# An attention and mixer kernel: transfers in another order with more buffers, the 1e-9 as a pair sum, other slots for key tiles and idle transposes

## The chip, the cores and the metric

One Trainium2 chip, of which the kernel uses one core. The metric is the device time in microseconds of one execution; the median of several runs is given. The engines are TensorE (PE; its weight loads are shown as PEld), VectorE (DVE), ScalarE (ACT), GpSimd (POOL), and SyncE (SP), which here only issues transfers. The engines run side by side, each works through its own instructions in order, and they wait for each other through semaphores.

## What is computed

Three stages, all in fp32 (`B, H, S, D = 2, 8, 768, 64`):

```python
# stage 1: attention over a window of 16 and over block summaries (block = 32)
k_sum = k.reshape(B, H, nb, block, D).max(axis=3)
v_sum = v.reshape(B, H, nb, block, D).mean(axis=3)
scores_l = scale * np.matmul(q, k.transpose(0, 1, 3, 2))      # kept where |i - j| < 16
scores_s = scale * np.einsum('bhsd,bhnd->bhsn', q, k_sum) + np.log(block)
a = np.exp(scores_all - np.max(scores_all, axis=-1, keepdims=True))
a = a / (np.sum(a, axis=-1, keepdims=True) + 1e-09)
x = np.matmul(a, np.concatenate([v, v_sum], axis=2))           # then (B, S, H*D)
# stage 2: h = relu(x @ w_in); u, v = halves; v normalised; u * (w_spatial @ v_n + b); @ w_out
# stage 3: h = relu(x @ w_in); conv of 3 taps over S; sigmoid gate; h * gate @ w_out
```

## The kernel before

Attention works on pairs of heads: 8 pairs, `p` = 0 to 7, and each pair in 3 groups of 4 query tiles of 64 (`GP = 3`, `GT = 4`), so `NG = 24` groups. A software pipeline runs over slots `i` = 0 to 28 (`SLOTS`). Every engine has its own loop over `i`; what is done for one group is spread over six slots:

- TensorE in slot `i`: `scores(i)` (L740, 16 small matmuls, waits for the maxima of group i-1, and at a new pair for the key tiles `kw` and for `q`); then the fills of the slot (`dense(u)`); then in slots under 17 without a `vs` fill four idle transposes (L845, they write a bank that nothing reads); then `transpose_probs(i-2)` (L750, waits for `norm_done` and for the `pT` copy of the group before); then `values(i-3)` (L763, at a new pair also waits for `v` and for the block sums in `vw`).
- VectorE: copy of `pT` of group i-3 (L589; for groups with n % 3 == 1 ScalarE does it, L490); in slots with i % 3 == 1 `key_maxima` of the next pair (L566); `x_l` of group i-5 (L597); for group i-1 `rinv`: add 1e-9 (L604), then the reciprocal (L606); for group i the mask, minimum and copy (L617, four pieces).
- ScalarE: `x_h` of group i-4 (L483), the `pT` copy where it is its turn, the four exponentials of group i (L495), whose accumulators write `rsum`, then the copies of the slot's fills.
- GpSimd, loop at L403: normalise group i-1 (L407, waits for `rinv`); `spread_windows` (L385) where i % 3 == 1, `spread_keys` (L377) where i % 3 == 2; then splitting of weights into a high and a low part (L368, L371): `parts` holds 18 such steps, 3 for each of 4 items `wi` and 2 items `wo`, and slots 3 to 16 take one, later ones two.

`key_maxima`, `spread_windows` and `spread_keys` of pair p+1 make the tiles that `scores(3(p+1))` needs.

The fills are units of other work that `fills_at` puts in slots. `("vs", p)` (L804, 24 small matmuls) and `("vp", p)` (L807, 2) make the block sums of `v`: `vs` in slot 3p-1, `vp` in slot 3p; ScalarE copies the result to `vsum`, and `load_sums(p)` spreads it into `vw`, which `values(3p)` reads. From slot 17 on, 14 fills of stage 2 for batch 0 (`("v", 0, m)`, `("u", 0, f, n)`) follow, 12 large matmuls each (`three`, L771 to L773). The first, `("v", 0, 0)`, waits for `wi_split` 8, the last of the 12 steps of the four `wi` items, and for x of batch 0. After the slots the rest of `seq` runs: batch 1, the product W, the spatial matmuls, then stage 3.

All transfers are issued by SyncE in one order written out by hand (L286 to L311): `load_k(p)`, `load_q(p)`, `load_v(p)`, `load_sums(p-1)`, an item (a weight tile, 512 KB) into one of three `stage` buffers. `k` has 2 buffers, `q` 2, `v` 3 (`NVB`). Each load first waits until its buffer is free (`ks_ready`, `win_pool`, `qk_done`, `pv_done`), and holds up what stands behind it.

`overlay` places tensors of different lifetimes in the same space of SBUF.

Of the kernel before, what the change touches and what calls it, by code (L numbers as in the profile page):

```python
# [19 lines left out]
BLOCK, WINDOW, TQ = 32, 16, 64  # L20


def attention_mixer_program(nc, qT_in, kT_in, vw_in, w_in, wsT_in, b_spatial, woT_in, w_in2, cw_in2, w_out2,
                            out):
    fp32 = mybir.dt.float32
# [26 lines left out]
    NVB, NP_, NST = 3, 4, 3  # L52
# [7 lines left out]
    WARM, KEEP = 20, 4  # L60
# [3 lines left out]
    with ctx:  # L64
# [6 lines left out]
        def overlay(name, *lives):  # L71

            found, most = [], 0
            for life in lives:
# [10 lines left out]
        kw, vw, vs_s, vsum, ks, W_h, W_l = overlay(  # L85
            "space_w",
            [("kw", [128, 2, NT, KA], fp32), ("vw", [KA, NVB, NT, 2 * D], fp32), ("vs_s", [128, 2, 2 * D], fp32),
             ("vsum", [128, 2, 2 * D], fp32), ("ks", [128, 2, NB], fp32)],
# [16 lines left out]
        vn0_h, vn0_l, uT0, _, vraw0, wo2_h, wo2_l = overlay(  # L105
            "space_v",
            [("vn0_h", [128, SC6, FH], f32r), ("vn0_l", [128, SC6, FH], f32r), ("uT0", [128, FC, S], fp32)],
            [("at_v0", [128, SC6, FH], fp32), ("vraw0", [128, SC6, FH], fp32)],
            [("wo2_h", [128, GC, DM], f32r), ("wo2_l", [128, GC, DM], f32r)])
        (qT, kT, P, pT, mask, asel, psel, w2_h, w2_l, woT_h, woT_l, g0_h, g0_l, g1_h, g1_l, _, gm0, _, gm1) = overlay(  # L110
            "space_a",
            [("qT", [128, 2, S], fp32), ("kT", [128, 2, S + 2 * WINDOW], fp32), ("P", [128, NP_, GT, KA], fp32), ("pT", [KA, 2, GT * 128], fp32),
# [15 lines left out]
        rsum = sb("rsum", [128, NG * GT], fp32)  # L128
# [14 lines left out]
        q_in = [sem(f"q_in{i}") for i in range(2)]  # L143
# [5 lines left out]
            sem("psel_ready"), sem("eps_ready"))  # L149
        ring_done, ks_ready, win_act, win_pool, kw_ready, vs_ready, vsum_ready = (  # L150
# [26 lines left out]
        for n, i in enumerate((17, 18, 19, 20, 21, 22, 23, 24, 24, 25, 25, 26, 27, 28)):  # L177
            fills_at[i].append(b0[n])
# [13 lines left out]
        def pT_count(n):  # L192

            return (pT_act, n // GP + 1) if n % GP == 1 else (pT_dve, n // GP * (GP - 1) + 1 + n % GP // 2)
# [53 lines left out]
        def _(sp):  # L248
# [6 lines left out]
            def load_q(p):  # L255
                if p >= 2:
                    sp.wait_ge(qk_done, GP * (p - 1))
                sp.dma_start(qT[:, p % 2, :], qT_in[p]).then_inc(q_in[p % 2], 16)
# [26 lines left out]

            load_k(0)  # L286
            load_q(0)
            load_v(0)
            load_k(1)
            load_q(1)  # L290
            load_v(1)
            load_sums(0)
            load_item(0)
            n = 1
            for p in range(2, NP):
# [3 lines left out]
                load_sums(p - 1)  # L299
# [3 lines left out]
            load_sums(NP - 1)  # L303
# [18 lines left out]
        def _(pool):  # L322
# [80 lines left out]
            for i in range(1, NG + 1):  # L403
# [5 lines left out]
                if i % GP == 1 and i // GP + 1 < NP:  # L409
                    spread_windows(i // GP + 1)  # L410
# [522 lines left out]
```

## Time and profile before

| | |
|---|---|
| median of 3 runs | 357.94 us (355.36 to 358.36) |
| the profiled execution | 356.37 us, of it the span 354.6 us |
| mean granted clock of TensorE | 0.995 |
| TensorE busy | 337.8 us, 95% of the span |
| VectorE busy | 212.5 us, 60% |
| ScalarE busy | 125.9 us, 35% |
| GpSimd busy | 113.1 us, 32% |
| chain that ended last, by engine | TensorE 84%, transfers 7%, ScalarE 3%, VectorE 2% |
| transfers | 25.85 MB; `v` 8 x 576 KB, `k` and `q` 8 x 384 KB each, block sums 8 x 144 KB |

The span goes from the first to the last instruction. A granted clock of 1.00 is 2.4 GHz and 0.50 is 1.2 GHz. The busy time of TensorE includes time in which a matmul is in flight behind another, so it is an upper bound of its work; the start of one group of matmuls to the start of the next is the better price.

### The profile page before, as it was taken

The numbers are of one execution on the slowest core, as the hardware profiler recorded it, in microseconds if no ns is written. First come the engines' busy times: TensorE is split into PE (matmuls) and PEld (weight loads), VectorE is DVE, ScalarE is ACT, GpSimd is POOL, SyncE is SP. The second block draws the span as 40 slices with busy tenths as digits, with TensorE's granted clock in tenths as the row PEclk, the third lists the DMA queues.
The fourth block names the chain that finished last, engine by engine and source line by source line (L and its number), as shares of the span: only waits on it lengthen the run. The fifth ranks groups of instructions, "written<-read, shape, count | busy, mean of one in ns | idle before, by whom it ended". The sixth has DMA issues, their size and how long they took to land.

```text
span 354.6 us, 6382 instructions
## 1 busy us (share of the span) xinstructions
PE 337.8 (95%) x2528; PEld 298.2 (84%) x2528; DVE 212.5 (60%) x498; ACT 125.9 (35%) x365; POOL 113.1 (32%) x124
## 2 busy tenths in 40 slices
PE   7859888999999999999999999999999999999996
PEld 6537566777999899888999999988888889999984
DVE  2558788534416992155345994678666557666652
ACT  4746677656434232253111114232222222222212
POOL 5577698822207999600001950000000000000000
PEclk9989999999999999999999999999999999999999
DMA  8696767502201310055000100000000004000004
GB/s 260 187 258 189 236 185 223 186 8 94 104 2 61 89 44 2 0 177 180 0 0 2 59 2 0 1 2 0 0 2 0 0 2 177 0 2 0 3 0 178
DMA packets 10526, 25.85 MB, mean 73 GB/s; under 512 B 1152, under 2 KB 3456, under 8 KB 10496
## 3 DMA queue, kind: packets, MB, share of 16 engines
q1 hardware_dynamic: 10496, 25.44, 23.0%
q8 instruction: 20, 0.33, 0.4%
q14 instruction: 10, 0.08, 0.1%
HBM read 21.11 MB, written 3.15 MB: 68 GB/s over the span
## 4 chain that ended last, share of the span: by engine, by line
PE 84%; DMA 7%; ACT 3%; DVE 2%; issue 1%; SPq 1%; POOL 0%; ACTq 0%; DVEq 0%
PE bank L771 26%; PE bank L773 25%; PE bank L772 25%; DMA kT<-in_k 4%; PE bank L763 3%; DMA vw<-in_vw 3%; ACT P L495 2%; PE bank L750 2%; PE bank L740 2%; PE bank L804 1%; DMA out<-obuf 1%; DVE rinv L604 1%; DVE ks L566 1%; DVE obuf L685 0%; DVE P L617 0%
## 5 line engine op out<-in xcount | busy, mean ns | idle before, releaser
L495 ACT ACTIVATE P<-P,nmax 128x120 f32<-128x120 f32 x96 | 36.7, 384 | 18.8 <-DVE nmax L617 18.7
L773 PE MATMUL bank<-g_h,W_l 128*128 128x384 f32 x128 | 43.0, 336 | 0.0
L772 PE MATMUL bank<-g_l,W_h 128*128 128x384 f32 x128 | 42.9, 335 | 0.0
L771 PE MATMUL bank<-g_h,W_h 128*128 128x384 f32 x128 | 42.9, 335 | 0.0
L773 PE MATMUL bank<-wo_h,hg_l 128*128 128x512 f32 x96 | 38.0, 396 | 0.0
L772 PE MATMUL bank<-wo_l,hg_h 128*128 128x512 f32 x96 | 38.0, 396 | 0.0
L771 PE MATMUL bank<-wo_h,hg_h 128*128 128x512 f32 x96 | 37.9, 395 | 0.0
L407 POOL TENSOR_TENSOR P<-P,rinv 128x480 f32<-128x480 f32 x24 | 23.7, 987 | 32.3 <-DVE rinv L606 32.3
L773 PE MATMUL bank<-wsT_h,vn_l 128*128 128x384 f32 x96 | 32.1, 334 | 0.0
L771 PE MATMUL bank<-wsT_h,vn_h 128*128 128x384 f32 x96 | 32.1, 334 | 0.0
L772 PE MATMUL bank<-wsT_l,vn_h 128*128 128x384 f32 x96 | 32.1, 334 | 0.0
L551 ACT ACTIVATE cbuf<-cbuf 128x768 f32<-128x768 f32 x16 | 13.5, 846 | 49.5 <-DVE cbuf L699 49.5
L542 ACT ACTIVATE hbuf<-bank 128x384 f32<-128x384 f32 x32 | 15.5, 490 | 41.0 <-PE bank L773 40.0
L589 DVE COPY pT<-bank 120x512 f32<-120x512 f32 x16 | 11.0, 690 | 27.3 <-PE bank L750 27.3
L617 DVE CUSTOM_DVE_ANT_0 P<-bank,mask 128x120 f32<-128x120 f32 x96 | 21.5, 278 | 8.1 <-PE bank L740 8.1
L710 DVE TENSOR_TENSOR pbuf<-hbuf,cbuf 128x768 f32<-128x768 f32 x16 | 15.3, 958 | 16.0 <-ACT cbuf L551 16.0
L771 PEld LDWEIGHTS bank<-g_h,W_h 128*128 128x128 f32 x128 | 24.0, 188 | 0.8 <-ACT hbuf L542 0.2
L772 PEld LDWEIGHTS bank<-g_l,W_h 128*128 128x128 f32 x128 | 24.0, 188 | 0.6
L773 PEld LDWEIGHTS bank<-g_h,W_l 128*128 128x128 f32 x128 | 24.0, 188 | 0.0
L524 ACT ACTIVATE g_h<-gm 128x384 fp32r<-128x384 f32 x16 | 8.4, 526 | 43.0 <-DVE gm L675 43.0
L694 DVE TENSOR_SCALAR cbuf<-hbuf,cw 128x768 f32<-128x768 f32 x16 | 9.9, 619 | 22.3 <-ACT hbuf L542 22.3
L771 PE MATMUL bank<-x_h,wi_h 128*128 128x384 f32 x64 | 22.0, 343 | 0.0
(107 smaller groups left out, 782.7 us busy)
## 6 DMA issues: line engine op xcount, KB each, us to landing
vw<-in_vw SPq DMA_DIRECT2D x8, 576.0 KB, 5.8
kT<-in_k SPq DMA_DIRECT2D x8, 384.0 KB, 5.0
qT<-in_q SPq DMA_DIRECT2D x8, 384.0 KB, 5.6
out<-obuf SPq DMA_DIRECT2D x12, 256.0 KB, 2.1
stage<-in_wsT SPq DMA_DIRECT2D x6, 384.0 KB, 3.0
stage<-in_w_in SPq DMA_DIRECT2D x4, 512.0 KB, 5.9
stage<-in_w SPq DMA_DIRECT2D x4, 512.0 KB, 5.0
stage<-in_wo SPq DMA_DIRECT2D x4, 512.0 KB, 3.6
```

What stands on the lines that cost most here:

```text
L407: g.tensor_tensor(out=pi, in0=pi, in1=rinv[:, n * GT:(n + 1) * GT].unsqueeze(2).to_broadcast([128, GT, KA]), op=ALU.mult).then_inc(norm_do ...
L495: a.activation(P[:, i % NP_, j, :], P[:, i % NP_, j, :], ACT.Exp, bias=nmax[:, c:c + 1], scale=-1.0, accum_out=rsum[:, c:c + 1]).then_inc( ...
L542: a.activation(hbuf[:, G % 2, 1 + n * HS:1 + (n + 1) * HS], bank[6 + n][:, 0:HS], ACT.Relu).then_inc(h_ready, 1)
L551: a.activation(cbuf[:, G % 2, :], cbuf[:, G % 2, :], ACT.Sigmoid).then_inc(sig_ready, 1)
L589: vv.tensor_copy(pT[:, n % 2, :], PTB[0:KA, :]).then_inc(pT_dve, 1)
L617: vv.tensor_tensor_reduce(out=P[:, i % NP_, j, :], in0=SC[e][:, h * KA:(h + 1) * KA], in1=mask[:, kind, :], scale=-SCALE, scalar=LARGEST, ...
L694: vv.tensor_scalar(c, h[:, 0:S], tap[0], None, ALU.mult).then_inc(conv_step, 1)
L710: vv.tensor_tensor(out=pbuf[:, :], in0=hbuf[:, G % 2, 1:S + 1], in1=cbuf[:, G % 2, :], op=ALU.mult).then_inc(hg_ready, 1)
L763: ins = t_.matmul(OT[i % 2][e * D:(e + 1) * D, j * TQ:(j + 1) * TQ], vw[:, p % NVB, r * GT + j, e * D:(e + 1) * D], pT[:, i % 2, (4 * e + ...
L771: t_.matmul(dst, lhs[0](c), rhs[0](c), start=first, stop=False)
L772: t_.matmul(dst, lhs[0](c), rhs[1](c), start=False, stop=False)
L773: ins = t_.matmul(dst, lhs[1](c), rhs[0](c), start=False, stop=last)
```

## The change

- `q` gets three buffers (`NQB`), `v` four (`NVB`). `kw` moves to another overlay to make room. The waits of `load_q` and `load_v` follow the new counts.
- SyncE's order: pairs 0 and 1 as before, then item 0, `k`(2), `q`(2), sums(0), item 1, `v`(2); then for p = 1 to 7: `k`(p+2), `v`(p+2), `q`(p+2), sums(p), an item.
- `rsum` becomes a pair for each column; the second is set to 1e-9 once, and `rinv` is made by a `tensor_reduce` over the pair instead of a `tensor_scalar` add.
- `key_maxima` and `spread_windows` of pair p+1 move from slot 3p+1 to 3p, `spread_keys` from 3p+2 to 3p+1 (for p = 0 they stay in slots 1, 1 and 2).
- ScalarE copies `pT` of the groups with n % 3 == 0 instead of 1.
- The splitting steps: none in slots under 2 and in slots 3p, one in other slots under 18, two from slot 18 on.
- The fills of batch 0 start in slot 18 and not 17; there are still 14, the last in slot 28.
- Warm-up transposes 17, not 20; idle transposes 4 in slots 0 to 2, 2 in later slots under 18 without fills, else none.

```diff
     HS = S // 2
-    NVB, NP_, NST = 3, 4, 3
+    NQB, NVB, NP_, NST = 3, 4, 4, 3
...
     QB = 3 * BLOCK // 16
-    WARM, KEEP = 20, 4
+    WARM = 17
     SLOTS = NG + 5
...
         nmax = sb("nmax", [128, NG * GT], fp32)
-        rsum = sb("rsum", [128, NG * GT], fp32)
+
+        rsum = sb("rsum", [128, NG * GT, 2], fp32)
         rinv = sb("rinv", [128, NG * GT], fp32)
...
         b0 = [("v", 0, m) for m in range(SC6)] + [("u", 0, f, n) for f in range(FC) for n in range(2)]
-        for n, i in enumerate((17, 18, 19, 20, 21, 22, 23, 24, 24, 25, 25, 26, 27, 28)):
+        for n, i in enumerate((18, 19, 20, 21, 22, 23, 24, 24, 25, 25, 26, 26, 27, 28)):
             fills_at[i].append(b0[n])
...
-            return (pT_act, n // GP + 1) if n % GP == 1 else (pT_dve, n // GP * (GP - 1) + 1 + n % GP // 2)
+            return (pT_act, n // GP + 1) if n % GP == 0 else (pT_dve, n // GP * (GP - 1) + n % GP)
...
             def load_q(p):
-                if p >= 2:
-                    sp.wait_ge(qk_done, GP * (p - 1))
-                sp.dma_start(qT[:, p % 2, :], qT_in[p]).then_inc(q_in[p % 2], 16)
+                if p >= NQB:
+                    sp.wait_ge(qk_done, GP * (p - NQB + 1))
+                sp.dma_start(qT[:, p % NQB, :], qT_in[p]).then_inc(q_in[p % NQB], 16)
...
-            load_k(0)
-            load_q(0)
-            load_v(0)
-            load_k(1)
-            load_q(1)
-            load_v(1)
-            load_sums(0)
-            load_item(0)
-            n = 1
-            for p in range(2, NP):
+            for p in range(2):
                 load_k(p)
...
                 load_v(p)
-                load_sums(p - 1)
+            load_item(0)
+            load_k(2)
+            load_q(2)
+            load_sums(0)
+            load_item(1)
+            load_v(2)
+            n = 2
+            for p in range(1, NP):
+                if p + 2 < NP:
+                    load_k(p + 2)
+                    load_v(p + 2)
+                    load_q(p + 2)
+                load_sums(p)
                 if n < 6:
...
                     n += 1
-            load_sums(NP - 1)
             sp.dma_start(cw[:, :], cw_in2).then_inc(cw_in, 16)
...
                                 op=ALU.mult).then_inc(norm_done, 1)
-                if i % GP == 1 and i // GP + 1 < NP:
+
+                if i == 1 or i >= GP and i % GP == 0 and i // GP + 1 < NP:
                     spread_windows(i // GP + 1)
-                if i % GP == 2 and i // GP + 1 < NP:
+                elif i == 2 or i >= GP and i % GP == 1 and i // GP + 1 < NP:
                     spread_keys(i // GP + 1)
-                for _ in range(0 if i < 3 else 1 if i < 17 else 2):
+                for _ in range(0 if i < 2 else 2 if i >= 18 else 0 if i % GP == 0 else 1):
                     if parts:
...
                                  ACT.Copy).then_inc(xh_ready, 1)
-                if 3 <= i < NG + 3 and (i - 3) % GP == 1:
+                if 3 <= i < NG + 3 and (i - 3) % GP == 0:
                     n = i - 3
...
                                      bias=nmax[:, c:c + 1], scale=-1.0,
-                                     accum_out=rsum[:, c:c + 1]).then_inc(exp_done, 1)
+                                     accum_out=rsum[:, c, 0:1]).then_inc(exp_done, 1)
                 for u in fills_at[i]:
...
             vv.memset(eps[:, :], 1e-6).then_inc(eps_ready, 1)
+            vv.memset(rsum[:, :, 1:2], 1e-9).then_inc(floor_ready, 1)
...
             for i in range(SLOTS):
-                if 3 <= i < NG + 3 and (i - 3) % GP != 1:
+                if 3 <= i < NG + 3 and (i - 3) % GP != 0:
                     n = i - 3
...
                     vv.tensor_copy(pT[:, n % 2, :], PTB[0:KA, :]).then_inc(pT_dve, 1)
-                if i % GP == 1 and i // GP + 1 < NP:
+                if i == 1 or i >= GP and i % GP == 0 and i // GP + 1 < NP:
                     key_maxima(i // GP + 1)
...
                     dve.wait_ge(exp_done, GT * i)
-                    vv.tensor_scalar(rinv[:, cols], rsum[:, cols], 1e-9, None, ALU.add).then_inc(den_ready, 1)
+                    if i == 1:
+                        dve.wait_ge(floor_ready, 1)
+                    vv.tensor_reduce(out=rinv[:, cols], in_=rsum[:, cols, :], op=ALU.add,
+                                     axis=AX.X).then_inc(den_ready, 1)
                     dve.wait_ge(den_ready, i)
...
                     pe.wait_ge(kw_ready, p + 1)
-                    pe.wait_ge(q_in[p % 2], 16 * (p // 2 + 1))
+                    pe.wait_ge(q_in[p % NQB], 16 * (p // NQB + 1))
                 if i >= 1:
...
                             ins = t_.matmul(SC[e][odd * TQ:(odd + 1) * TQ, h * KA:(h + 1) * KA],
-                                            qT[rows, p % 2, t * TQ:(t + 1) * TQ], kw[rows, p % 2, t, :],
+                                            qT[rows, p % NQB, t * TQ:(t + 1) * TQ], kw[rows, p % 2, t, :],
                                             start=True, stop=True)
...
                     dense(u)
-                if i < 17 and not any(u[0] == "vs" for u in fills_at[i]):
-                    for _ in range(KEEP):
-                        t_.transpose(bank[2][:, 0:128], ident[:, :], ident[:, :])
+                for _ in range(4 if i < 3 else 2 if i < 18 and not fills_at[i] else 0):
+                    t_.transpose(bank[2][:, 0:128], ident[:, :], ident[:, :])
                 if 2 <= i < NG + 2:
...
                 if 3 <= i < NG + 3:

```

## Rows read from the trace of the kernel before

**Rows 1.** Stretches: length, busy PE, PEld, DVE, ACT, POOL, clock, DMA share, GB/s

```profile
61.78:354.60 292.82, 289.49 (x1716) 261.72 (x1712) 171.61 (x298) 86.17 (x195) 67.79 (x59) 1.00 0.13 42
```

**Rows 2.** Chain of waits up to 66 us: start us, duration us, what

```profile
14.82 8.91 DMA vw<-in_vw
23.77 1.51 PE bank L804 x24
...
27.36 0.61 PE bank L740 x16
...
31.79 8.01 DMA kT<-in_k
```

**Rows 3.** Stretches of the attention slots, columns as in rows 1

```profile
2.00:12.00 10.00, 8.06 (x102) 6.46 (x104) 4.04 (x21) 5.06 (x21) 5.96 (x17) 1.00 0.87 273
...
14.00:27.00 13.00, 8.81 (x140) 6.45 (x141) 6.23 (x36) 7.00 (x32) 7.86 (x8) 0.88 0.93 266
27.00:61.00 34.00, 28.73 (x535) 21.54 (x531) 28.11 (x135) 24.93 (x111) 28.10 (x29) 1.00 0.70 208
...
24.00:25.00 1.00, 1.00 (x24) 0.78 (x16) 0.00 (x0) 0.00 (x0) 1.00 (x2) 0.50 1.08 412
```

**Rows 4.** Timeline of TensorE: start us, duration, engine, line, tiles, shape, count

```profile
36.12 0.40 PE L807 MATMUL bank<-vs_s,psel 128*24 128x128 f32 x2
36.45 0.66 PE L845 MATMUL bank<-ident 128*128 128x128 f32 x4
36.94 0.60 PE L750 MATMUL bank<-ident,P 128*120 128x128 f32 x4
37.47 0.69 PE L763 MATMUL bank<-pT,vw 120*64 120x64 f32 x16
38.09 0.64 PE L740 MATMUL bank<-kw,qT 64*64 64x120 f32 x16
...
60.41 0.64 PE L740 MATMUL bank<-kw,qT 64*64 64x120 f32 x16
60.98 0.86 PE L804 MATMUL bank<-vw,asel 96*32 96x128 f32 x24
61.78 0.50 PE L771 MATMUL bank<-wi_h,x_h 128*128 128x512 f32 x1
```

**Rows 5.** Timeline of VectorE, columns as in rows 4

```profile
18.16 0.95 DVE L566 TENSOR_REDUCE ks<-kT 128x24 f32<-128x768 f32 x1 [2.69 <-DMA kT<-in_k]
...
49.44 0.28 DVE L617 CUSTOM_DVE_ANT_0 P<-bank,mask 128x120 f32<-128x120 f32 x1
...
51.78 1.12 DVE L604 TENSOR_SCALAR rinv<-rsum 128x4 f32<-128x4 f32 x1
...
53.05 0.28 DVE L617 CUSTOM_DVE_ANT_0 P<-bank,mask 128x120 f32<-128x120 f32 x1
...
55.26 0.54 DVE L604 TENSOR_SCALAR rinv<-rsum 128x4 f32<-128x4 f32 x1
...
55.96 0.28 DVE L617 CUSTOM_DVE_ANT_0 P<-bank,mask 128x120 f32<-128x120 f32 x1
...
58.28 0.28 DVE L617 CUSTOM_DVE_ANT_0 P<-bank,mask 128x120 f32<-128x120 f32 x1
```

**Rows 6.** Instructions of L604 and L566: duration ns least/median/most, first and last start

```profile
L604 DVE TENSOR_SCALAR rinv<-rsum x24: 157/170/1121, 9.6 to 94.5; 128x4 f32<-128x4 f32 x24
...
L566 DVE TENSOR_REDUCE ks<-kT x8: 946/951/954, 3.9 to 67.3; 128x24 f32<-128x768 f32 x8
```

**Rows 7.** Timeline of GpSimd, columns as in rows 4

```profile
50.50 1.14 POOL L385 COPY kw<-kT 128x1152 f32<-128x1152 f32 x1
51.60 1.27 POOL L371 TENSOR_TENSOR wi_l<-stage,wi_h 128x512 fp32r<-128x512 f32 x1
53.19 0.99 POOL L407 TENSOR_TENSOR P<-P,rinv 128x480 f32<-128x480 f32 x1 [0.32 <-DVE rinv L606]
```

**Rows 8.** Timeline of SyncE, the issue of k of pair 2

```profile
13.75 0.55 SPq L253 DMA_DIRECT2D kT<-in_k  x1
```

More of the change, by code:

```diff
@@ L83, in overlay @@
             return found
-        kw, vw, vs_s, vsum, ks, W_h, W_l = overlay(
+        vw, vs_s, vsum, ks, W_h, W_l = overlay(
             "space_w",
-            [("kw", [128, 2, NT, KA], fp32), ("vw", [KA, NVB, NT, 2 * D], fp32), ("vs_s", [128, 2, 2 * D], fp32),
-             ("vsum", [128, 2, 2 * D], fp32), ("ks", [128, 2, NB], fp32)],
+            [("vw", [KA, NVB, NT, 2 * D], fp32), ("vs_s", [128, 2, 2 * D], fp32), ("vsum", [128, 2, 2 * D], fp32),
+             ("ks", [128, 2, NB], fp32)],
             [("W_h", [128, FC, FF], f32r), ("W_l", [128, FC, FF], f32r)])
@@ L104, in attention_mixer_program @@
             [("at_v1", [128, SC6, FH], fp32), ("vraw1", [128, SC6, FH], fp32)])
-        vn0_h, vn0_l, uT0, _, vraw0, wo2_h, wo2_l = overlay(
+        vn0_h, vn0_l, uT0, _, vraw0, kw, wo2_h, wo2_l = overlay(
             "space_v",
@@ L108, in attention_mixer_program @@
             [("at_v0", [128, SC6, FH], fp32), ("vraw0", [128, SC6, FH], fp32)],
+            [("kw", [128, 2, NT, KA], fp32)],
             [("wo2_h", [128, GC, DM], f32r), ("wo2_l", [128, GC, DM], f32r)])
@@ L111, in attention_mixer_program @@
             "space_a",
-            [("qT", [128, 2, S], fp32), ("kT", [128, 2, S + 2 * WINDOW], fp32), ("P", [128, NP_, GT, KA], fp32), ("pT", [KA, 2, GT * 128], fp32),
+            [("qT", [128, NQB, S], fp32), ("kT", [128, 2, S + 2 * WINDOW], fp32), ("P", [128, NP_, GT, KA], fp32), ("pT", [KA, 2, GT * 128], fp32),
              ("mask", [128, 3, KA], fp32), ("asel", [KW, 3, 32], fp32), ("psel", [128, 4, QB], fp32)],
@@ L142, in attention_mixer_program @@
         k_in = [sem(f"k_in{i}") for i in range(2)]
-        q_in = [sem(f"q_in{i}") for i in range(2)]
+        q_in = [sem(f"q_in{i}") for i in range(NQB)]
         v_in = [sem(f"v_in{i}") for i in range(NVB)]
@@ L149, in attention_mixer_program @@
             sem("psel_ready"), sem("eps_ready"))
+        floor_ready = sem("floor_ready")
         ring_done, ks_ready, win_act, win_pool, kw_ready, vs_ready, vsum_ready = (
```

## The prediction

> **What bounds the kernel now.** I read the stretches first. From 61.78 us to the end TensorE is busy for 289.49 of 292.82 us [rows 1], and what is left is a few missing records and the tail. That is the dense work, from the first fill `("v",0,0)` on; attention is hidden behind it from slot 17 on. Everything that the change touches acts before 61.78, or moves work across that line. So the question is when the first dense fill starts, and how much TensorE work stands behind it.
>
> Before that line the chain of waits is made of transfers and small work [rows 2]: `v` of pair 2 lands at 14.82+8.91 = 23.73 us, and another piece is `k` of a later pair, 8.01 us up to 39.80. The transfer engines are nearly full from 14 to 27 us (share 0.93, 266 GB/s), and 0.70 full from 27 to 61 us [rows 3]. I write s(i) for the scores of slot i and P(i) for the start of its first L617. The PE timeline shows what one slot costs TensorE [rows 4]: scores 0.57 (60.41 to 60.98), a `vs` fill 0.80, a `vp` fill 0.33 (36.12 to 36.45), four idle transposes 0.49, the transposes of P 0.53, the values 0.61.
>
> **The pace without transfers.** P(i) needs the exp of slot i-1 and then `rinv`. From P(13) at 49.44 to the start of L604 at 51.78 is 2.34, and 0.32 follows if L604 is short: 2.66. From 53.05 to 55.26+0.32 is 2.53, from 55.96 to 58.28 is 2.32 [rows 5]. That is 7.5 for three slots; the first record after 53.05 follows after 0.5 instead of 0.2, once, so I take 7.4. The first of the three is long because ScalarE copies a `pT` there; the change moves that copy to another slot of the three and keeps it. As it ran, the same three slots took 58.28-49.44 = 8.84.
>
> **The change, part by part.**
>
> 1. The 1e-9 as a pair sum. L604 takes 157 ns at best, 1121 at worst [rows 6]. Its longest instance runs from 51.78 to 52.90, and GpSimd's L371 from 51.60 to 52.87 [rows 5, 7]: it ends as GpSimd's instruction ends. A `tensor_reduce` stands in the trace as L566, 768 elements a partition: 946 to 954 ns in all eight, whatever GpSimd did [rows 6]. So I cost the new reduce of 8 elements between 0.16 (the short L604; nothing added) and 0.95 (L566), and take 0.17 because it is nearest to the small one. This gives the 7.4 a cycle instead of up to 8.84. The Trainium skill ("SBUF — State Buffer", Who interferes with whom) says that a `tensor_scalar` in a two-port mode and GpSimd shut each other out, and that `tensor_reduce` never contends on trn2; the trace agrees, with 1.12 us against a steady 0.95. Against it speaks "VectorE: DVE Perf Modes" (The perf-mode tier table), by which `tensor_reduce` runs at 1x where fp32 `tensor_scalar` runs at 2x; on 8 elements that would add nearly nothing, on L566's size half a microsecond.
>
> 2. Key tiles one slot earlier, no split in slots 3p. GpSimd now does normalise 0.99, windows 1.10 (50.50 to 51.60) and a split 1.27 in one slot [rows 7], 3.4 us against a pace of 2.47, and s(3p) waits for the keys behind it. After, 3p holds 0.99+1.10, the next slot keys and a split, and the keys have two slots of slack. Cost nothing; hidden behind ScalarE's exp.
>
> 3. But one split in three is dropped. `wi` has 12 parts. Before they are done in GpSimd's slots 3 to 14. After, the slots with a part are 2, 4, 5, 7, 8, 10, 11, 13, 14, 16, 17: eleven. **The twelfth comes in slot 18, behind the normalise and the windows, and `("v",0,0)`, now in TensorE's slot 18, waits for all twelve.** TensorE is in order: transposes, values and s(19) stand behind it. The fill can start at P(18) + 0.14 (to GpSimd, 53.05 to 53.19) + 0.99 + 1.10 + 1.27 = P(18)+3.5, that is P(17)+2.66+3.5 = P(17)+6.2. TensorE would be free after the four pieces of P(17), s(18) and `vp`: P(17)+0.85+0.57+0.33 = P(17)+1.8. That is a stall of 4.4 us. A shorter stall, the wait for `v` up to 23.77, was followed by the lower clock: 0.50, that is 1.2 GHz, in 24 to 25 us, the `vs` fill taking 1.51 [rows 2, 3]. By s(6) at 27.36, whose scores took their usual 0.61, it was over, some 3.4 us; half of that, 1.7 us, I charge again here. The skill's "TensorE: Matmul & The Clock Gate" (HAM oscillation) describes such a drop after a wait for a transfer; the trace agrees, with the 0.50.
>
> 4. The fill moves from slot 17 to 18. Before, 354.6-61.78 = 292.8 follow the start of the first fill. After, the transposes and values of slot 17, s(18) and `vp` come ahead of it: 0.53+0.61+0.57+0.33 = 2.04. So 290.8 follow.
>
> 5. Idle transposes. Plain slots have 2, not 4 (-0.25), `vp` slots none (-0.49), slots 0 and 2 gain 0.49 each. TensorE's slots are then 1.96, 2.04 and 2.5 us, under the 2.47 pace on average, so this frees little; the 0.49 in slots 0 and 2 stand beside waits for `v` and are free. Three fewer warm-up transposes end before slot 0, whose exps wait behind nothing, but slot 1 is set by `v`(0) and `k`(1): nothing. The extra memset of `rsum` lies in VectorE's first wait: nothing.
>
> 6. Transfers. All go through SP's queue, in order. Item 0 goes out at about 4 us instead of 13, `k`(2) and `q`(2) follow at once (before, `k`(2) went out at 13.75, behind sums(0) and item 0 [rows 8]), sums(0) and item 1 after them, then `v`(2). Rate at a full share: 273/0.87 = 314, 266/0.93 = 286, 208/0.70 = 297 GB/s [rows 3]; I take 300. So `k` or `q` (0.393 MB) is 1.3 us, `v` 2.0, an item 1.75, the sums 0.5. The first six end at 2+0.87x10 = 10.7. Then item 0 12.45, `k`(2) 13.8, `q`(2) 15.1, sums(0) 15.6, item 1 17.3, `v`(2) 19.3, `k`(3) 20.6, `v`(3) 22.6, `q`(3) 23.9, sums(1) 24.4. Landing is later than this reckoning: `k`(2) was used at 18.16 [rows 5] where the bytes from 13.9 on give 17.0 (1.1 late), `v`(2) landed at 23.73 where they give 20.2 (3.5 late).
>    - Slot 3 needs `k`(2): 13.8+1.1 = 14.9, key maxima 0.87, then 0.32: P(3) = 16.1.
>    - Slot 5's `vs` fill needs `v`(2): between 20.4 and 22.8, I take 21.7. Then 0.80+0.53+0.61, scores 0.64, 0.07: P(6) = 24.4; by the pace alone 16.1+7.4 = 23.5. Before, s(6) ran at 27.36 and P(6) behind it at 28.1, so some 3.7 us are won here.
>    - Slot 6's values need sums(1): 25.5 to 27.9, I take 26.7. Then P(7) = 26.7+0.61+0.71 = 28.0 instead of 24.4+2.5 = 26.9: 1.1 late (0 to 2.3). This is what is late next: the sums now queue behind `k`(3), `v`(3), `q`(3).
>    - Later cycles: one pair is 1.3+1.3+2.0+0.5+1.75 = 6.85 us of transfer against 7.4 of pace, issued a cycle and more ahead; the waits for `k`(4) and `q`(4) go.
>
> **The sum.** P(18) = 24.4 + 4x7.4 + 1.1 = 55.1. First fill 58.6. End 58.6+290.8+1.7 = 351.1, against 354.6: -3.5 us. The profiled execution took 356.37, its span and 1.77 around it; the median is 357.94. From the median: **354.4 us** (a profiled execution by itself 356.37-3.5 = 352.9).
>
> **Rivals.**
> - *The sums and `v` land on time and the stall stays cheap* (0.12). P(6) 23.5, no delay in slot 7, no low clock: 23.5+29.6+3.5+290.8 = 347.4, -7.2: 350.7 us. For it: the reckoned ends 19.3 and 24.4. Against: 3.5 us late for `v`(2).
> - *The transfers stay the bound* (0.25). If every pair's share is as slow as landing shows, with the queue never empty, each of the four cycles after slot 6 loses 0.8 us (7.4 to 8.2) and the 3.5 is eaten: 357.6. For it: share 0.93 in 14 to 27 us, and the deeper queue ahead of each sums. Against: 0.70 in 27 to 61.
> - *Slower: the clock falls in the slots* (0.10). Fewer idle transposes leave TensorE thinner. At the low level the `vs` fill is 1.51 instead of 0.86, a slot about 3.9 instead of 2.47 [rows 2, 4]. Each slot at 1.2 GHz costs some 1.45 us, so it decides from the third slot on; five slots give 354.4+7.2 = 361.6. Against: from 27 to 61 us TensorE was busy 28.73 of 34 us and the clock stayed 1.00 [rows 3]; thinner slots at a faster pace are about as busy, 2.2 of 2.47.
> - *The reduce waits for GpSimd as L604 did* (0.05): cycles of 8.2 to 8.8, 357.6 to 360.
> - My own case 0.48.
>
> **Range and chances.** In my case P(6) may be 23.5 to 25.5 (-0.9, +1.1), the wait for sums 0 to 2.3 (-1.1, +1.2) and four cycles 7.3 to 7.5 (-0.4, +0.4): 352.0 to 357.1. To hold 8 in 10 the range takes in the first two rivals: 350.5 to 358.5. A measurement of this kernel tells about 1% (3.6 us) from no change. Faster by more: the first rival and half of my own case with a bit of the second, 0.40; within 1%: 0.49; slower: 0.11.
>
> **What would show it.** L604's successor at a steady 0.16 to 0.2 us; three-slot cycles near 7.4 from slot 7 on; `vs` of slot 5 starting near 21.7; values of slot 6 held for sums(1); TensorE idle about 4 us ahead of the first dense matmul with GpSimd's L371 as releaser and the clock at 0.5 after it; first dense matmul near 58.6 and 291 to 293 us behind it. Wrong if the first dense matmul is before 56 or after 61, if the clock falls between slots 7 and 17, or if the dense part has new gaps.

## The result, and the profile after

| | before | changed |
|---|---|---|
| median | 355.62 us (20 runs, 354.52 to 358.68) | 359.84 us (20 runs, 357.31 to 362.89) |
| ratio | | 1.0092, 95% interval 1.0068 to 1.0117 |
| profiled execution: span | 354.6 us | 357.1 us |
| first dense fill starts | 61.78 us | 64.79 us |

The changed kernel is 0.9% slower. I forecast 354.4 us with a range up to 358.5: the sign was wrong and the time lies outside. The chip runs some executions in a slower state; the ratio is over the fast ones alone, while the medians in the table are over all (they give 1.012).

The stretch behind the first dense fill (columns as in [rows 1]) is as forecast. It answers to [rows 1]:

```profile
64.79:357.10 292.31, 288.96 (x1674) 261.31 (x1674) 168.13 (x277) 81.60 (x175) 66.50 (x57) 0.99 0.11 36
```

292.3 us against the 290.8+1.7 of the sum. All but 0.2 us of what was missed lies ahead of 64.79. The chain of waits of the changed kernel in that part, start and duration, answers to [rows 2]:

```profile
18.91 8.84 DMA vw<-vsum
27.99 1.06 PE bank L773 x16
29.06 1.01 PE bank L750 x16
...
37.62 7.93 DMA vw<-vsum
45.79 1.12 PE bank L773 x16
46.91 1.01 PE bank L750 x16
```

The two long pieces of before, `v` of pair 2 and `k` of pair 4, are gone. In their place stand the block sums: issued at 18.91 and 37.62, landed 8.8 and 7.9 us later, and the scores behind each wait take 1.01 us where they took 0.61. The timeline of TensorE (start, duration, what, idle time before it) gives the waits:

```profile
7.75 1.51 PE L814 MATMUL bank<-vw,asel 96*32 96x128 f32 x24 [1.18 <-DMA vw<-in_vw]
...
23.17 0.64 PE L750 MATMUL bank<-kw,qT 64*64 64x120 f32 x16
...
27.99 1.06 PE L773 MATMUL bank<-pT,vw 120*64 120x64 f32 x16 [3.06 <-DMA vw<-vsum]
...
45.79 1.12 PE L773 MATMUL bank<-pT,vw 120*64 120x64 f32 x16 [1.91 <-DMA vw<-vsum]
...
60.50 0.64 PE L750 MATMUL bank<-kw,qT 64*64 64x120 f32 x16
61.15 0.40 PE L817 MATMUL bank<-vs_s,psel 128*24 128x128 f32 x2
64.79 0.50 PE L781 MATMUL bank<-wi_h,x_h 128*128 128x512 f32 x1 [3.24 <-POOL wi_l L376]
```

As in the prediction, s(i) is the scores of slot i and P(i) the start of VectorE's first mask instruction of slot i. s(6) starts at 23.17, where before it ran at 27.29 (27.36 in the chain of [rows 2]): 4.1 us ahead. s(17) starts at 57.94 against 60.41: 2.5 ahead. s(18) follows at 60.50. Then the first fill waits 3.24 us for GpSimd and is 3.0 behind. The ledger of the span: +3.01 for the fill's start, -2.04 for the work that moved ahead of it, and +1.5 that is left over behind it. I put this last part down to the low clock there: it was granted at 0.69 from 64.79 to 67 and at 0.50 from 67 to 69, and a_split below, without that wait, needs 1.7 us less behind its first fill. Together +2.5, and 357.1-354.6 = 2.5. (These are the two profiled executions; the ratio makes it 3.3.)

GpSimd's timeline is the chain that I wrote down for slot 18, link by link (rows of before: [rows 7]):

```profile
61.44 0.99 POOL L412 TENSOR_TENSOR P<-P,rinv 128x480 f32<-128x480 f32 x1
62.37 1.14 POOL L390 COPY kw<-kT 128x1152 f32<-128x1152 f32 x1
63.47 1.26 POOL L376 TENSOR_TENSOR wi_l<-stage,wi_h 128x512 fp32r<-128x512 f32 x1
```

The new add, the pair sum at L613, is short in all 24 cases (rows of before: [rows 6]; nanoseconds, least, median, most):

```profile
L613 DVE TENSOR_REDUCE rinv<-rsum x24: 149/152/165, 9.6 to 92.6; 128x4 f32<-128x8 f32 x24
```

And the transfers, by stretch (last three columns: granted clock, share, GB/s; rows of before: [rows 3]):

```profile
2.00:12.00 10.00, 8.81 (x80) 6.58 (x79) 3.67 (x19) 3.66 (x13) 5.94 (x17) 1.00 1.00 321
...
14.00:27.00 13.00, 10.26 (x190) 7.53 (x186) 10.63 (x58) 11.03 (x49) 11.71 (x13) 1.00 0.92 255
27.00:60.00 33.00, 29.10 (x509) 22.15 (x511) 22.94 (x129) 23.31 (x104) 22.61 (x25) 0.84 0.90 228
```

From 27 to 60 us the share is 0.90 and not 0.70, for 228 GB/s and not 208: at a full share 253 GB/s. From 15 to 50 us the share is 0.99, at the same 253 GB/s. The sum had used 300. The clock of this stretch is 0.84, where it was 1.00. Cut finer around the second wait (43.88 to 45.79), it shows where the clock goes:

```profile
39.00:42.00 3.00, 3.00 (x80) 2.34 (x78) 2.82 (x14) 2.59 (x14) 3.00 (x4) 1.00 0.91 193
42.00:45.70 3.70, 1.44 (x22) 0.75 (x16) 2.71 (x16) 2.90 (x14) 2.85 (x4) 0.93 1.00 290
45.70:48.00 2.30, 2.21 (x33) 1.82 (x34) 0.01 (x1) 0.38 (x1) 2.18 (x3) 0.50 1.01 208
48.00:50.00 2.00, 2.00 (x18) 1.66 (x20) 1.46 (x9) 1.62 (x8) 0.00 (x0) 0.50 0.96 200
50.00:53.00 3.00, 3.00 (x54) 2.20 (x50) 2.18 (x13) 1.54 (x8) 2.19 (x2) 0.67 0.28 63
```

TensorE is busy for all of 39 to 42 at 1.00; it works 1.44 of the next 3.7 us, and behind the wait it runs at 0.50, which is 1.2 GHz, until about 52 (the `vs` fill at 51.38 still takes 1.14 us, the transposes at 52.45 again 0.65). The same happens behind the first wait: 0.50 from 29 to 31.

### The profile page after: what moved, and what is told of

Its sections match the earlier page's. It is cut to its first block, busy times and chain, and to the rows that moved or that the text cites. A ratio compares the mean times of both kernels' runs of the same rounds, so it can differ in the third digit from the quotient of the medians.

```text
span 357.1 us, 6333 instructions
## 1 busy us (share of the span) xinstructions
PE 341.1 (96%) x2503; PEld 300.3 (84%) x2503; DVE 208.4 (58%) x499; ACT 126.0 (35%) x365; POOL 112.9 (32%) x124
## 4 chain that ended last, share of the span: by engine, by line
PE 86%; DMA 7%; POOL 2%; ACT 2%; DVE 1%; issue 0%; SPq 0%; DVEq 0%; POOLq 0%
PE bank L781 26%; PE bank L782 25%; PE bank L783 25%; DMA vw<-vsum 5%; PE bank L773 3%; PE bank L750 3%; PE bank L760 2%; DMA vw<-in_vw 2%; ACT P L501 1%; PE bank L814 1%; PE bank L854 1%; POOL P L412 1%; POOL wi_l L376 1%; DMA out<-obuf 1%; DVE obuf L695 0%
## 5 line engine op out<-in xcount | busy, mean ns | idle before, releaser
L412 POOL TENSOR_TENSOR P<-P,rinv 128x480 f32<-128x480 f32 x24 | 23.7, 987 | 32.1 <-DVE rinv L616 31.9
L720 DVE TENSOR_TENSOR pbuf<-hbuf,cbuf 128x768 f32<-128x768 f32 x16 | 15.3, 958 | 15.9 <-ACT cbuf L557 15.9
L781 PE MATMUL bank<-wi_h,x_h 128*128 128x512 f32 x48 | 20.1, 418 | 3.2 <-POOL wi_l L376 3.2
```

What stands on the lines that cost most here:

```text
L412: g.tensor_tensor(out=pi, in0=pi, in1=rinv[:, n * GT:(n + 1) * GT].unsqueeze(2).to_broadcast([128, GT, KA]), op=ALU.mult).then_inc(norm_do ...
L720: vv.tensor_tensor(out=pbuf[:, :], in0=hbuf[:, G % 2, 1:S + 1], in1=cbuf[:, G % 2, :], op=ALU.mult).then_inc(hg_ready, 1)
L781: t_.matmul(dst, lhs[0](c), rhs[0](c), start=first, stop=False)
```

## The experiments

All ratios are to the kernel before, run beside them, with the 95% interval behind; the changed kernel stands at 1.0092 (1.0068 to 1.0117). Runs whose label begins with a_ start from the changed kernel, those with b_ from the kernel before, split_actq and those with ss_ from the changed kernel with repairs. Times inside an execution are those of the one that was profiled, and differences of 1 or 2 us in the first slots come and go between executions of kernels that are alike there.

**The splitting steps.**

```diff
-                for _ in range(0 if i < 2 else 2 if i >= 18 else 0 if i % GP == 0 else 1):
+                for _ in range(0 if i < 2 else 2 if i >= 18 else 0 if i % GP == 0 and i < 12 else 1):
```

> The changed kernel with a splitting step also in slots 12 and 15, so that the twelfth is done by slot 16. Theory B (the first dense fill waits for the twelfth step, 3.24 us, and pays 1.5 us of low clock after it): both go, the fill starts at about 61.6 instead of 64.8 and the time falls by 4 to 5 us, ratio to before about 0.997. Rival (the fill would wait for something else, or the two extra steps hold up the key tiles of slots 12 and 15 as in the kernel before): it falls by less than 2 us.

Measured: 0.9957 (0.9930 to 0.9984), 1.35% less than the changed kernel, 4.8 us. The fill stands directly behind `vp`:

```profile
60.62 0.64 PE L750 MATMUL bank<-kw,qT 64*64 64x120 f32 x16
61.26 0.40 PE L817 MATMUL bank<-vs_s,psel 128*24 128x128 f32 x2
61.59 0.50 PE L781 MATMUL bank<-wi_h,x_h 128*128 128x512 f32 x1
```

s(18) is where it was (60.62, 60.50). The fill starts 3.20 us sooner, and behind it stand 352.2-61.59 = 290.6 us instead of 292.3. The wait of 3.24 us and the low clock behind it come from the steps left out in slots 12 and 15. Theory B holds. (Ahead of slot 18 the two executions are not alike: s(6) was 1.2 us later and the slots from there 1.0 us shorter, with waits for the sums in both.)

**The block sums ahead of v and q.**

```diff
                     load_k(p + 2)
+                load_sums(p)
+                if p + 2 < NP:
                     load_v(p + 2)
                     load_q(p + 2)
-                load_sums(p)
```

> The changed kernel with the block sums of pair p issued ahead of v and q of pair p+2. Theory C (values of slots 6 and 12 wait 3.1 and 1.9 us for sums that queue behind v and q, and the clock falls after each): both waits go, slots 7 and 13 to 14 run at 2.4 GHz, scores of slot 18 start 5 to 7 us earlier than 60.50, and the time falls by as much, ratio about 0.993. Rival (the transfer engines are full and something else is late in its place, v or k of the next pair): the wait moves to a vs fill or to the key maxima and the time falls by less than 2 us.

Measured: 0.9978 (0.9948 to 1.0008), 1.14% less than the changed kernel, 4.1 us. No values wait for the sums any more; what is left for `v` and `k` sits in the first slots. s(6) is at 27.02 and s(18) at 55.71: 28.7 us for 12 slots, where the changed kernel took 60.50-23.17 = 37.3. The sums are issued as long before their use as in the changed kernel, but with only `k` of the new pair ahead of them. Issue of the sums of pair 3 and the start of the values that read them, without a wait:

```profile
37.26 0.82 SPq L268 DMA_DIRECT2D vw<-vsum  x1
...
43.33 0.69 PE L774 MATMUL bank<-pT,vw 120*64 120x64 f32 x16
```

So they landed in less than 6.1 us, where they took 7.9 and 8.8. Clock and share of the stretch:

```profile
27.00:57.00 30.00, 28.23 (x564) 21.00 (x562) 26.60 (x149) 27.28 (x123) 26.62 (x29) 0.99 0.91 275
```

So the two waits cost 8.6 us by slot 18: 3.06+1.91 of waiting, and the other 3.7 I put down to the slots at 1.2 GHz. Each of the four cycles of three slots now takes 7.2 us, for the same bytes: the amount to be moved did not forbid that pace. Not all of the 8.6 is seen in the profiled execution: `v` of pairs 0 and 2 came late (TensorE waited 2.72 us for the one and 1.80 for the other) and s(6) ran 3.9 us later than in the changed kernel's, and the fill, which still waits for GpSimd, starts 4.8 us sooner, at 59.99. The order of issue up to `v` of pair 2 is the same in both kernels, so the edit is not what made those two late.

**Both.**

The two diffs together.

> The changed kernel with both repairs: splitting steps also in slots 12 and 15, and the block sums issued ahead of v and q. Alone they gave 0.9957 and 0.9978 against the kernel before, the changed kernel 1.0092. If the two losses are separate, as the traces say (one acts in slots 6 and 12, one in slot 18), the gains add: 1.0092 - 0.0135 - 0.0114 = 0.984, some 350 us, first dense fill near 56.5. Rival (the transfer engines set the time of slot 18 once both are gone): not under 0.992.

Measured: 0.9798 (0.9751 to 0.9844), median 350.66 us against 356.1. It beats both kernels. The gains add: 1.0092-0.0135-0.0114 = 0.984 lies at the edge of the interval, so that there was something on top is not shown. The timeline at slot 18:

```profile
53.63 0.64 PE L751 MATMUL bank<-kw,qT 64*64 64x120 f32 x16
54.27 0.40 PE L818 MATMUL bank<-vs_s,psel 128*24 128x128 f32 x2
54.59 0.50 PE L782 MATMUL bank<-wi_h,x_h 128*128 128x512 f32 x1
```

The first fill at 54.59, 7.2 us ahead of before.

**The pair sum alone**, in the kernel before.

```diff
-        rsum = sb("rsum", [128, NG * GT], fp32)
+        rsum = sb("rsum", [128, NG * GT, 2], fp32)
...
-                                     accum_out=rsum[:, c:c + 1]).then_inc(exp_done, 1)
+                                     accum_out=rsum[:, c, 0:1]).then_inc(exp_done, 1)
...
+            vv.memset(rsum[:, :, 1:2], 1e-9).then_inc(floor_ready, 1)
...
-                    vv.tensor_scalar(rinv[:, cols], rsum[:, cols], 1e-9, None, ALU.add).then_inc(den_ready, 1)
+                    if i == 1:
+                        dve.wait_ge(floor_ready, 1)
+                    vv.tensor_reduce(out=rinv[:, cols], in_=rsum[:, cols, :], op=ALU.add,
+                                     axis=AX.X).then_inc(den_ready, 1)
```

> The kernel before with only the pair sum. Theory D (the short reduce does not wait for GpSimd): 0.15 to 0.19 us in all 24, three-slot cycles without a transfer wait of 7.5 instead of 8.9 us. As the waits for k and v of the kernel before stay and absorb most of it, the time falls by 0.5 to 3 us, ratio 0.992 to 0.999. Rival (what is won is fully given back at the next transfer): 1.000.

Measured: 0.9914 (0.9880 to 0.9948), first fill at 57.58 instead of 61.78; the reduce takes 148 to 163 ns. This one change is worth 0.9%, at the upper end of what was expected. Theory D holds for the instruction: it no longer waits for GpSimd. The pace did not come out as expected: three slots without a wait for a transfer (s(9) at 33.82 to s(12) at 41.79) took 8.0 us and not 7.5. How the gain splits is not shown: of the 4.2 us by which the fill starts sooner, 1.8 are there at s(6) (25.50 against 27.29), behind a shorter wait for `v` of pair 2.

**The new transfers alone, and all but the new transfers.**

The buffers, their places and the order of the change, in the kernel before (its core):

```diff
-    NVB, NP_, NST = 3, 4, 3
+    NQB, NVB, NP_, NST = 3, 4, 4, 3
...
-                load_sums(p - 1)
+            load_item(0)
+            load_k(2)
+            load_q(2)
+            load_sums(0)
+            load_item(1)
+            load_v(2)
+            n = 2
+            for p in range(1, NP):
+                if p + 2 < NP:
+                    load_k(p + 2)
+                    load_v(p + 2)
+                    load_q(p + 2)
+                load_sums(p)
...
```

> The kernel before with only the new order of transfers and the buffers (3 for q, 4 for v, kw in the other overlay). The changed kernel with the old transfers took 1.0428, so there the new transfers were worth 3.4%. If that worth is their own, this one lands at 0.97 to 0.985. If it came only from the key tiles having moved a slot ahead (which need k earlier), this one is at 0.995 to 1.005: v of pair 2 comes in time, but the sums of slots 6 and 12 wait as in the changed kernel.

Measured: 0.9987 (0.9935 to 1.0038).

The reverse, in the changed kernel, with the order of loads of the kernel before:

```diff
-    NQB, NVB, NP_, NST = 3, 4, 4, 3
+    NQB, NVB, NP_, NST = 2, 3, 4, 3
...
-                if p + 2 < NP:
-                    load_k(p + 2)
-                    load_v(p + 2)
-                    load_q(p + 2)
-                load_sums(p)
+                load_sums(p - 1)
...
```

> The changed kernel with the transfers' order and the buffer counts of the kernel before (2 for q, 3 for v); all else as changed. If the new order and depth are the loss (transfers share 0.90 at 253 GB/s instead of 0.70), the time falls below the changed kernel by 2 us or more, ratio to before 1.003 or less. If they are a gain that the rest eats (I forecast 3.7 us won by slot 6), it rises by 2 us or more, ratio 1.015. The long waits of before for v of pair 2 and k of pair 4 should come back in it either way.

Measured: 1.0428 (1.0393 to 1.0463). The two do not contradict each other. By themselves the new transfers give nothing: in that kernel's chain of waits stand other transfers, `v` of pair 1 and the sums of pair 1, and not shorter ones than before. (The profiled execution took 360.75 us, 2.9 above its median, so it shows which waits there are and not how long they are as a rule.)

```profile
3.14 12.77 DMA vw<-in_vw
...
21.85 12.55 DMA vw<-vsum
```

But key maxima a slot earlier in VectorE's queue need them. With the old order VectorE stands at L571 for `k`, and everything behind it on that engine with it (waits: total us, times, longest):

```profile
DVE ks L571 <- DMA kT<-in_k: 21.9, 7, 4.8
```

In the same stretch of the trace, 10 to 75 us, VectorE waited for `k` 4.8 us in two waits in the kernel before, and in the changed kernel hardly at all:

```profile
DVE ks L573 <- DMA kT<-in_k: 0.2, 1, 0.2
```

I had put the move of the key tiles down as free; with `k` late it is not. That these waits are the larger part of the 3.4% between a_old_transfers and the changed kernel is likely and was not tested by itself.

**The rest: key tiles, splitting, idle transposes, fills from slot 18.** The run b_pair_new_sums has the pair sum, new transfers and sums first in the kernel before (the three diffs above put together). It lacks the moved key tiles and ScalarE's moved `pT` copy, the new slots of splitting steps, idle transposes and fills, and the shorter warm-up:

> The kernel before with three parts: the pair sum, the new transfers, and the sums issued ahead of v and q. Not in it: key tiles a slot earlier, the other splitting and idle transposes, the fills from slot 18. If the moved key tiles and the fewer splitting steps are worth something by themselves (theory F), it stays 1% or more behind the repaired changed kernel (0.9798), at 0.990. Rival: 0.980, and all the gain is in these three parts.

Measured: 0.9897 (0.9839 to 0.9955), 1% behind the repaired changed kernel (0.9751 to 0.9844). The intervals just touch; theory F is likely, not certain, and which of the parts left out it would be stays open.

Two more undo one part each in the repaired kernel of a_split_sums. The idle transposes:

```diff
-                for _ in range(4 if i < 3 else 2 if i < 18 and not fills_at[i] else 0):
+                for _ in range(4 if i < 17 and not any(u[0] == "vs" for u in fills_at[i]) else 0):
```

> The repaired changed kernel (0.9798) with the idle transposes of the kernel before: four in every slot under 17 without a vs fill. Theory G (fewer idle transposes cost nothing and save 0.25 to 0.49 us of TensorE where it is not the limit): 0.979 to 0.984. Rival (they keep the clock up, my slower rival of the prediction): the low clock of the first 12 us goes and it is 0.973 or less.

Measured: 0.9839 (0.9793 to 0.9884). With the idle transposes of before the first vs fill still waited for `v` up to 9.37, and s(6) to s(18) took 29.75 instead of 29.30 us. The interval overlaps that of the kernel without them, and the medians are alike (350.77 and 350.66 us): as theory G has it, they do not pay for themselves. The low clock of the first 12 us is still there with them (that `vs` fill takes 1.51 us), so their absence isn't what lowered it; behind the waits for the sums this was not tried.

The slots of the fills:

```diff
-        for n, i in enumerate((18, 19, 20, 21, 22, 23, 24, 24, 25, 25, 26, 26, 27, 28)):
+        for n, i in enumerate((17, 18, 19, 20, 21, 22, 23, 24, 24, 25, 25, 26, 27, 28)):
```

> The repaired changed kernel with the first dense fill back in slot 17. It has all twelve splitting steps by slot 16, and the rows of x by then. TensorE has pauses up to slot 18 which the fill covers: 0.3 to 1 us less, 0.977 to 0.979. Rival (the fill in slot 17 pushes s(18) and with it the last key tiles later, dense work is the limit from there anyhow): no difference.

Measured: 0.9827 (0.9775 to 0.9880), no difference that shows, as the rival had it; I had expected 0.3 to 1 us less. The twelfth step is then the limit again: the fill in slot 17 waited 1.6 us for it.

**The warm-up.**

```diff
-    WARM = 17
+    WARM = 20
```

> The changed kernel with 20 warm-up transposes instead of 17. Theory A (the three transposes left out keep TensorE at 1.2 GHz in the first slots): the first vs fill takes 0.86 us instead of 1.51, scores of slot 3 start near 13.9 instead of 15.93, and the time falls by 1 to 2 us against the changed kernel (ratio to before about 1.005 instead of 1.009). Rival (the low clock at the start is chance, or its loss is swallowed by the later waits for the block sums): the first slots change or not, the time stays within 0.5 us of the changed kernel.

Measured: 1.0118 (1.0075 to 1.0162).

```diff
-    WARM, KEEP = 20, 4
+    WARM, KEEP = 17, 4
```

> The kernel before with 17 warm-up transposes instead of 20. Theory A (three fewer leave the first slots at 1.2 GHz, scores of slot 3 some 2 us later): 1.003 to 1.006. Rival, which the changed kernel with 20 speaks for (it did not get faster, and its first vs fill waited for v up to 9.4 us): no difference, 0.998 to 1.002, and the level of the first 12 us changes from run to run with the arrival of v of pair 0.

Measured: 1.0009 (0.9978 to 1.0040). Theory A falls: three more transposes give nothing back, three fewer cost nothing clear of the noise (0.4% at most). The first scores took 0.64 us in a_warm20 and 1.08 in the changed kernel, but 0.95 with 20 transposes and 0.90 with 17 in the other pair, so even there the number alone decides nothing. Behind them the wait for `v` of pair 0 brings the low clock, with 20 transposes too (timeline of TensorE in a_warm20):

```profile
5.57 0.64 PE L750 MATMUL bank<-kw,qT 64*64 64x120 f32 x16
9.40 1.51 PE L814 MATMUL bank<-vw,asel 96*32 96x128 f32 x24 [3.19 <-DMA vw<-in_vw]
```

**Why the sums land so late.** Four runs. Theory E is that transfers issued behind the sums hold them up, theory H that their small pieces do.

```diff
                 load_sums(p)
+                sp.wait_ge(vw_ready[p % 2], 16 * (p // 2 + 1))
```

> The changed kernel in which SyncE, having issued the sums of a pair, issues nothing more until they have landed. Theory E (a transfer shares the engines with those issued after it): in the changed kernel sums(1) landed when 7.61 MB had moved though only 6.84 MB had been issued up to it, sums(3) at 12.0 of 10.94 MB. With nothing behind them they land at 6.8 to 7.0 and 10.9 to 11.1 MB, 5 to 6.5 us after their issue instead of 9.1 and 8.0, and the values of slots 6 and 12 wait 1 to 3 us less. Rival (transfers land in the order of issue and only the rate is low): the sums land 8 to 9 us after their issue as before.

Measured: 1.0232 (1.0172 to 1.0293). Theory E falls. With nothing issued behind them the sums of pair 1 landed no sooner:

```profile
23.03 10.30 DMA vw<-vsum
```

The bytes came out as expected (219 GB/s x 31.3 us = 6.85 MB at the landing), which with nothing issued behind them they had to; the time did not. The stretches of one us up to there show how such a queue ends (clock, share, GB/s are the last three):

```profile
29.00:30.00 1.00, 0.99 (x22) 0.54 (x18) 1.00 (x2) 0.86 (x2) 0.00 (x0) 1.00 0.86 183
30.00:31.00 1.00, 0.63 (x4) 0.41 (x4) 0.96 (x10) 0.32 (x3) 0.50 (x1) 1.00 0.31 59
31.00:32.00 1.00, 0.00 (x0) 0.00 (x0) 1.00 (x6) 1.00 (x7) 1.00 (x2) 1.00 0.13 39
32.00:33.00 1.00, 0.00 (x0) 0.00 (x0) 0.54 (x3) 0.58 (x3) 0.78 (x2) 1.00 0.07 23
```

The last 3 us have shares of 0.31, 0.13 and 0.07, as much as five, two and one of the 16 engines busy all the time. The sums landed only at the end of this tail.

```diff
-                sp.dma_start(vw[KW:KA, p % NVB, :, :],
-                             vsum[KW:KA, p % 2, :].unsqueeze(1).to_broadcast([NB, NT, 2 * D])).then_inc(vw_ready[p % 2], 16)
+                sp.dma_start(vw[KW:KA, p % NVB, :, :], vw_in[p][0:NB]).then_inc(vw_ready[p % 2], 16)
```

> The changed kernel in which the block sums' place is filled from the first 24 rows of the v windows in HBM: the same bytes at the same point of the queue, but one piece of 6 KB a partition instead of 12 of 512 B out of SBUF. It leaves out the block sums' part of the output. Theory H (the small pieces are what is slow: the last 2 to 3 us of a queue that runs dry have a share of 0.07 to 0.28): the transfers' share ends at once, the rate at a full share from 27 to 45 us goes from 250 to 290 GB/s or more, the waits of slots 6 and 12 (3.06, 1.91 us) shrink by half or more, and the time falls by 2 to 5 us. Rival (the sums only stand behind 1.5 to 2 MB of other transfers): landing 7 us or more after the issue as before, time within 1.5 us of the changed kernel.

This kernel leaves out the block sums' part of the output; only its timing counts. Measured: 1.0068 (1.0031 to 1.0104), against 1.0092 for the changed kernel; the intervals overlap. The transfer in the sums' place in pair 1 was issued at 20.55 and landed 11.86 us later, with 232 GB/s at a full share from 27 to 45 us. Theory H falls: it isn't the small pieces.

```diff
-            load_sums(0)
...
-                load_sums(p)
...
+                    act.wait_ge(vsum_ready, p + 1)
+                    if p >= NVB:
+                        act.wait_ge(pv_done, GP * (p - NVB + 1))
+                    act.dma_start(vw[KW:KA, p % NVB, :, :],
+                                  vsum[KW:KA, p % 2, :].unsqueeze(1).to_broadcast([NB, NT, 2 * D])).then_inc(vw_ready[p % 2], 16)
```

> The changed kernel with the sums issued by ScalarE right behind its copy, through its own queue, in place of SyncE's. Rival of H (it is the place in the queue): they land 3 to 4 us after their issue, the values of slots 6 and 12 wait for nothing, and the clock stays up there. ScalarE pays 0.5 to 0.9 us of issue a pair, in slot 3p, which is on the path: 8 x 0.7, of which 5 count, 3.5 us. Together 2 to 4 us less than the changed kernel, ratio 1.000. By theory H they would still land 6 us or more after the issue and the time would rise above the changed kernel.

Measured: 1.0215 (1.0150 to 1.0280). Its own queue gave the sums no lead: those of pair 0 took 12.50 us, and TensorE waited 8.01 us for them in slot 3:

```profile
15.10 12.50 DMA vw<-vsum
```

Behind that late start no values waited for sums in slot 6, as the expectation had it, but that says little. And the run changes two things: SyncE no longer stops for the sums, so an item and `v` of pair 2 (6.01, 6.49) and `k` and `v` of pair 3 (13.73, 14.11) were issued ahead of the sums of pair 0, and not behind them. Bytes issued less bytes moved (286 GB/s from 2 to 15.1 us) leave some 2.4 MB open at their issue, an estimate; in the changed kernel it is some 0.2 MB (4.06 MB issued, 332 GB/s from 2 to 13.65). What the run shows is that 0.15 MB in another queue did not pass 2.4 MB.

The same with the splitting steps of a_split.

> The same with splitting steps also in slots 12 and 15. If a_actq ends near 1.000, this one gains the 1.3% of the splitting steps on top, 0.986; the other repair, the sums ahead of v and q in SyncE's own queue, gave 0.9798 and should stay the better one, because it costs ScalarE nothing.

Measured: 1.0111 (1.0065 to 1.0156), better than a_actq by the worth of the splitting steps (1.04%), and 3% behind a_split_sums. The sums of pair 0 took 13.71 us here (15.88 to 29.59), the longest of all runs.

So: where TensorE waited for it under a full share, the small transfer took 6.4 to 13.7 us from issue to landing, in SyncE's queue or another, in small pieces or large; behind `k` alone it took less than 6.1. It is needed some 6 us after it can be issued, so what counts is what has been issued ahead of it. The tail in a_hold suggests that the engines are loaded unevenly; that is argued, and which transfers would cause it was not tried and stays open.

## Why the prediction was wrong, by its own steps

- **Pair sum**: right. 0.15 us (I took 0.17), and worth 0.9% by itself. By the Trainium skill ("SBUF — State Buffer", Who interferes with whom) a `tensor_reduce` never contends with GpSimd on trn2; the trace agrees, with 149 to 165 ns in all 24. The 1x rate that the Trainium skill ("VectorE: DVE Perf Modes", The perf-mode tier table) gives for it costs nothing that shows on 8 elements (a median of 152 ns against 170 for the `tensor_scalar`).
- **Pace without transfers**: 7.4 us for three slots was forecast; the clean cycle from s(9) at 34.65 to s(12) at 41.80 took 7.15. Right, a little cautious. In a_sums_first it was 7.2, in b_pair, without the moved key tiles, 8.0.
- **The twelfth splitting step**: right in place and nearly in size. The stall was 3.24 us, not 4.4: TensorE was free only at P(17)+2.6 (58.98 to 61.55), because s(18) stands behind the `vs` fill, transposes and values of slot 17, which my P(17)+1.8 left out, and P(18) came 2.3 and not 2.66 behind P(17). The fill stands at P(18)+3.5 as forecast (61.30, 64.79). The low clock after it cost 1.5 to 1.7 (1.7). a_split shows it.
- **Fill moved by a slot**: right, 292.3 behind it against 292.5.
- **Slots 3 to 6**: s(6) at 23.17, where the working gives 23.7.
- **First wait for sums**: right in kind, too small in price. They landed at 27.75 (I took 26.7, range up to 27.9). I charged 1.1 us and no low clock, although I charged one for the stall in slot 18. The wait of 3.06 us is longer than the one that lowered the clock in the kernel before:

```profile
23.77 1.51 PE L804 MATMUL bank<-vw,asel 96*32 96x128 f32 x24 [2.84 <-DMA vw<-in_vw]
```

  From s(6) to s(12) the changed kernel took 18.6 us, and the sum has 2x7.4+1.1 = 15.9: 2.7 us missed here.
- **Later cycles: the step that failed.** "One pair is 6.85 us of transfer against 7.4 of pace, issued a cycle and more ahead", so no wait was charged from slot 7 on. Two things in it do not hold. First, the sums cannot be issued a cycle ahead. They exist only after `vp` of slot 3p and are read in slot 3p+3: issued at 18.91 and 37.62, needed at 24.93 and 43.88 (where TensorE's waits begin), 6.0 and 6.3 us later. Behind `k`, `v` and `q` of a later pair they took 8.8 and 7.9. Second, the 300 GB/s came from stretches in which the queue was short or ran dry. From 15 to 50 us, at a share of 0.99, it was 253 GB/s, so a pair takes 2.05 MB/0.253 = 8.1 us, more than the pace, and the queue did not empty. The wait of slot 12 (1.91 us) with its low clock was not in the sum at all: s(12) to s(18) took 18.7 us against 14.8, 3.9 missed. With the 2.7 of the first wait, less the 0.5 won by s(6), that is the 6.1 us by which s(18) came later than forecast (60.50 against 55.1-0.7 = 54.4). a_sums_first shows the cause: with the sums ahead of `v` and `q` both waits are gone. It shows too that of the two errors the place in the queue is the one that decides, since the same bytes went through at 7.2 us a cycle. Why the sums landed later than the bytes ahead of them would give stays open (those of pair 1 landed when 294 GB/s x 25.9 us = 7.61 MB had moved, with 6.85 MB issued up to them).
- **Rivals.** The second one, "the transfers stay the bound", came nearest: a deeper queue ahead of each of the sums, and a share near 1. It had 0.25 and should have been the first, since the bytes per pair over the lowest of the three rates in [rows 3] already gave 7.2 us against 7.4, hardly a margin. But its 357.6 us is no change against the 357.94 that it was reckoned from, and its cycle of 8.2 us was 9.3: it has neither the waits nor the clock, and by a_sums_first the transfers did not bound the cycle by their amount. The slower rival named the clock too, but from thin slots; the clock fell behind waits.
- **Signs of being wrong.** Two of the three that I named came: the first dense matmul after 61, and the clock falling between slots 7 and 17.
- **Idle transposes, warm-up**: costed at nothing, and no difference was measured. **Key tiles a slot earlier**: costed at nothing; with the old order of transfers it is not (a_old_transfers).

## What to carry to other kernels

Take the rate for a queue that you make deeper from a stretch in which it never runs dry, and where the transfers of a cycle come near the cycle (here 6.85 us by the sum and 8.1 as measured, against 7.4), order the queue by due time: the small transfer that is issued last and needed first goes ahead of the large ones. Count its lead from the moment at which its data exist, which here was 6 us. When work is thinned out over slots, count the steps up to the first consumer; one step of 1.3 us that came in slot 18, where before it came in slot 14, cost 4.8 us. And a wait of TensorE of 2 to 3 us cost here its own length and most of that again in slots at 1.2 GHz.

## What the hardware showed that I had not expected

- A transfer of 0.15 MB behind others under a full share took 7.9 and 8.8 us from issue to landing in the changed kernel, 10.30 with nothing behind it (a_hold), 11.86 in large pieces (a_sums_rows), and 12.50 and 13.71 through another engine's queue (a_actq, split_actq).
- A queue that ran dry needed 3 us for its tail, at shares of 0.31, 0.13 and 0.07.
- At a full share the rate ran from 232 GB/s (a_sums_rows, 27 to 45 us) over 253 (changed kernel, 15 to 50 us) to 321 (changed kernel, 2 to 12 us).
- Behind a wait of 1.91 us the clock was at 1.2 GHz: it was granted at 1.00 up to 42 and at 0.50 from 45.7, and the chain has the scores behind the wait at 1.01 us.
